# A kernel of attention and three MLP stages: X is turned for the token stage by VectorE and small transfers in place of TensorE

## The chip, the cores and the metric

The kernel runs on one core of a Trainium2 chip. The metric is the device time of one execution in microseconds (us). Engines are TensorE (PE), VectorE (DVE), ScalarE (ACT), GpSimd (POOL) and SyncE (SP), which here only issues transfers (DMA). SBUF is the on-chip memory of 128 partitions, PSUM the accumulators that PE writes; PE can't write SBUF.

## The reference, cut to what matters

There are 4 batches of S = 576 tokens with 512 features. Three stages follow one another:

```
x = attention(q, k, v)                       # 8 heads of 64, windowed and dilated masks
xk, xr = mu * x + (1 - mu) * x_prev          # feed-forward with token shift
x = sigmoid(xr @ w_r) * (relu(xk @ w_k)**2 @ w_v)
xt = x.transpose(0, 2, 1)                    # token mixer
u  = x + (relu(xt @ w_tok1) @ w_tok2).transpose(0, 2, 1)      # w_tok1 576x256
out = u + relu(u @ w_ch1) @ w_ch2            # channel mixer, w_ch1 512x1536
```

All matrices are float32. A product is made of three PE passes on two parts of each operand: hi (the value rounded to fp32r, by ACT) and lo (value minus hi, by DVE or POOL): hi*hi, lo*hi and hi*lo (lines 761 to 763).

## The kernel before, in words

Everything is kept with features on the partitions: `X` holds for each batch 4 blocks of 128 features, each 577 columns (tokens) wide, and is computed in phase 1 (attention and feed-forward, interleaved by tables of units: `ff[t]` is the list of steps of unit t, 20 units for each half batch, counted from the end with negative numbers). Phase 2 does the token mixer and the channel mixer, batch after batch.

The token mixer's first product, `token_up` (L1104), contracts over tokens, so it needs x with tokens on the partitions: `xT`, 5 tiles of 512 features, four of 128 tokens and a tail of 64 tokens, the tail written twice, to both halves of the partitions. `x_transpose` (L1061) makes it: for a tile, PE does 4 transposes by a product with `ident` (L1082) into a PSUM bank, ACT rounds the bank to `xT_hi` (L1093, L1094) and DVE subtracts to `xT_lo` (L1100, L1101). For batch 0 these steps stand in the last two half batches of the feed-forward, two units apart. For batches 1 to 3 they stand near the end of the channel mixer of the batch before, behind its last `channel_up` (`if i == len(seq)` in `phase2_body`), because `xT` shares its memory with `u`, the operand of `channel_up`. They read `xcur`, a copy of the batch's X that POOL requests (`load_x`, L1030).

In the channel mixer 24 steps (2 halves of 288 tokens, 12 blocks of 128 of the 1536) each do `channel_up` (12 matmuls into one of four `work` banks), ACT's `h_hi` and DVE's `h_lo`, and, two steps later, `channel_down` (12 matmuls into four accumulators). `ORDER` and `READ` say which of the four work banks a product gets and whose reading it must wait for. Output: `finish` adds, `out_blocks` (DVE, STREAM_TRANSPOSE, which turns each 32x32 block in place) and `store` (SP, 16 transfers of 32 partitions for each half batch, in runs of 32 floats).

Each engine executes its own list in order, and all waits are on semaphores. SP's list is: loads of q, k, v and weights; `load_token_weights`; `load_channel_weights`; then the stores of each batch.

## Time and profile before

| | before |
|---|---|
| median of 3 runs | 729.09 us (728.98 to 730.18) |
| the profiled execution's own time | 729.79 us |
| its span, first to last instruction | 728.0 us |
| PE, DVE, ACT, POOL busy | 715.6, 372.6, 255.9, 224.8 us |

PE is the engine with almost no idle time in any part. In a row of the timeline the first number is the start in us, the second the duration in us, then engine, line, operation, output<-input, shapes and how many instructions were merged; in square brackets stands the idle time before it and what ended that. Matmuls overlap in PE's pipeline, so the distance of their starts tells their price, not the duration.

### The profile page before, as it was taken

What the parts mean: (1) busy time and instruction counts of PE and PEld (TensorE: products, weight loads), DVE (VectorE), ACT (ScalarE), POOL (GpSimd) and SP (SyncE); (2) the same over time, 40 slices, a digit from 0 to 9 for tenths busy, and PEclk for the clock granted to TensorE, in tenths of its full rate; (3) what the DMA queues carried; (4) which work ended last, traced back from release to release, by engine and by line L of the source; (5) the groups of instructions that cost most, each with busy time, mean ns of one, the idle gap of its engine ahead of it and who ended that gap; (6) DMA issues with size and microseconds to landing.
All of it is one profiled execution on the core that took longest, in us unless ns stands there. A gap on an engine that the chain in (4) does not pass through costs nothing.

```text
span 728.0 us, 15646 instructions
## 1 busy us (share of the span) xinstructions
PE 715.6 (98%) x6463; PEld 691.6 (95%) x6463; DVE 372.6 (51%) x629; ACT 255.9 (35%) x628; POOL 224.8 (31%) x237
## 2 busy tenths in 40 slices
PE   8999999999999999999999999999999999999997
PEld 7778899999999999999999998999999999999997
DVE  6588877687777768576741224412244122451222
ACT  3585463635454453645431112311123111231111
POOL 5497664756464655734054000000000000000000
PEclk9999999999999999999999999999999999999999
DMA  9921333222322320201902011200103002010021
GB/s 210 295 60 31 53 72 69 48 56 50 73 39 50 66 41 20 70 1 36 375 2 66 6 29 19 80 1 1 33 14 85 1 1 33 9 25 1 1 34 33
DMA packets 127190, 39.89 MB, mean 55 GB/s; under 512 B 116168, under 2 KB 120720, under 8 KB 127120
## 3 DMA queue, kind: packets, MB, share of 16 engines
q1 hardware_dynamic: 122864, 33.39, 20.5%
q0 software_dynamic: 1088, 4.72, 1.9%
q10 hardware_dynamic: 3168, 0.79, 0.6%
q8 instruction: 51, 0.84, 0.5%
q14 instruction: 19, 0.16, 0.1%
HBM read 29.43 MB, written 4.72 MB: 47 GB/s over the span
## 4 chain that ended last, share of the span: by engine, by line
PE 90%; DVE 3%; POOL 2%; issue 1%; DMA 1%; ACT 1%; DVEq 0%; POOLq 0%; ACTq 0%
PE bank L761 12%; PE bank L763 11%; PE bank L762 11%; PE tq L761 8%; PE tq L762 8%; PE tq L763 8%; PE bank L1245 4%; PE bank L1244 4%; PE s L1245 4%; PE bank L1243 4%; PE s L1243 3%; PE s L1244 3%; PE bank L683 3%; PE s L549 2%; PE bank L647 1%
## 5 line engine op out<-in xcount | busy, mean ns | idle before, releaser
L1220 DVE SCALAR_TENSOR_TENSOR h_lo<-tq,h_hi 128x288 fp32r<-128x288 f32 x48 | 22.0, 457 | 114.1 <-ACT h_hi L1216 114.1
L1220 DVE SCALAR_TENSOR_TENSOR h_lo<-bank,h_hi 128x288 fp32r<-128x288 f32 x48 | 22.0, 458 | 113.4 <-ACT h_hi L1216 113.4
L881 DVE RECIPROCAL rg<-rg 128x288 f32<-128x288 f32 x32 | 61.2, 1919 | 3.0 <-ACT rg L870 3.0
L1216 ACT ACTIVATE h_hi<-tq 128x288 fp32r<-128x288 f32 x48 | 19.7, 411 | 122.3 <-PE tq L763 122.3
L1216 ACT ACTIVATE h_hi<-bank 128x288 fp32r<-128x288 f32 x48 | 19.7, 411 | 121.7 <-PE bank L763 121.7
L848 POOL TENSOR_TENSOR k_lo<-kr,k_hi 128x288 fp32r<-128x288 f32 x64 | 54.5, 857 | 24.8 <-ACT k_hi L844 23.9
L1035 POOL DMA_DIRECT2D xcur<-X x4 | 3.2, 798 | 180.4 <-DVE U L1162 163.8
L1245 PE MATMUL bank<-h_lo,C_hi 128*128 128x288 f32 x192 | 56.9, 296 | 0.0
L1244 PE MATMUL bank<-h_hi,C_lo 128*128 128x288 f32 x192 | 56.9, 296 | 0.0
L1243 PE MATMUL s<-h_hi,C_hi 128*128 128x288 f32 x192 | 56.9, 296 | 0.0
L1245 PE MATMUL s<-h_lo,C_hi 128*128 128x288 f32 x192 | 56.8, 296 | 0.0
L1243 PE MATMUL bank<-h_hi,C_hi 128*128 128x288 f32 x192 | 56.8, 296 | 0.0
L1244 PE MATMUL s<-h_hi,C_lo 128*128 128x288 f32 x192 | 56.7, 295 | 0.0
L761 PE MATMUL bank<-u_hi,C_hi 128*128 128x288 f32 x192 | 56.7, 295 | 0.0
L761 PE MATMUL tq<-u_hi,C_hi 128*128 128x288 f32 x192 | 56.6, 295 | 0.0
L762 PE MATMUL tq<-u_hi,C_lo 128*128 128x288 f32 x192 | 56.6, 295 | 0.0
L762 PE MATMUL bank<-u_hi,C_lo 128*128 128x288 f32 x192 | 56.6, 295 | 0.0
L763 PE MATMUL tq<-u_lo,C_hi 128*128 128x288 f32 x192 | 56.6, 295 | 0.0
L763 PE MATMUL bank<-u_lo,C_hi 128*128 128x288 f32 x192 | 56.6, 295 | 0.0
L761 PE MATMUL bank<-k_hi,WV_hi 128*128 128x288 f32 x184 | 55.8, 304 | 0.0
L762 PE MATMUL bank<-k_hi,WV_lo 128*128 128x288 f32 x184 | 54.3, 295 | 0.0
L763 PE MATMUL bank<-k_lo,WV_hi 128*128 128x288 f32 x184 | 54.1, 294 | 0.0
(215 smaller groups left out, 2241.1 us busy)
## 6 DMA issues: line engine op xcount, KB each, us to landing
C_raw<-in_moe_w_ch SPq DMA_DIRECT2D x6, 1024.0 KB, 11.6
xcur<-X POOLq DMA_DIRECT2D x4, 1152.0 KB, 5.8
out_x<-blocks SPq DMA_DIRECT2D x112, 36.0 KB, 1.7
vt<-in_v SPq DMA_DIRECT2D x40, 80.0 KB, 2.5
qraw<-in_q SPq DMA_DIRECT2D x128, 24.0 KB, 1.9
kraw<-in_k SPq DMA_DIRECT2D x128, 24.0 KB, 1.9
vt<-in_v SPq DMA_DIRECT2D x7, 320.0 KB, 3.4
WK_raw<-in_moe_w_k SPq DMA_DIRECT2D x4, 512.0 KB, 7.3
```

The costliest lines, as they stand in the source:

```text
L549: last = e.matmul(s2[64 * a:64 * a + 64, c0:c0 + KB], qT[rows, q0:q0 + 64], keys(rows, s, c), start=True, stop=True)
L683: last = e.matmul(o_[64 * h:64 * h + 64, SU * s + QB * c:SU * s + QB * (c + 1)], raw_v(n, slice(0, KB), 2 * s + h)[:, D * c:D * (c + 1)], ...
L761: e.matmul(out_ap, wh, xh, start=start and i == 0, stop=False)
L762: e.matmul(out_ap, wl, xh, start=False, stop=False)
L763: last = e.matmul(out_ap, wh, xl, start=False, stop=stop and i == len(kts) - 1)
L848: e.tensor_tensor(lo, t, hi.bitcast(F32), ALU.subtract).then_inc(Z.lo_done, 1)
L881: e.reciprocal(t, t).then_inc(Z.r_done, 1)
L1216: e.activation(hi, ps, ACT.Relu).then_inc(Z.h2h_done, 1)
L1220: e.scalar_tensor_tensor(lo, ps, 0.0, hi.bitcast(F32), ALU.max, ALU.subtract).then_inc(Z.h2l_done, 1)
L1243: e.matmul(o_, wh, xh, start=f == 0, stop=False)
L1244: e.matmul(o_, wl, xh, start=False, stop=False)
L1245: return e.matmul(o_, wh, xl, start=False, stop=f == FT2 - 1)
```

## The change

`x_transpose` is gone. In its place:

- `x_blocks(b, d)`: DVE turns the 32x32 blocks of feature block d of batch b in `X` into a buffer `xblocks` (one instruction for the four full token tiles, one for the tail). For b > 0 it waits for the stores of batch b - 2 and the copy of batch b - 1, since `xblocks` lies on memory that they read.
- `x_rows(b)`: SP issues 32 transfers from SBUF to SBUF that carry the blocks to their rows: 16 for the tail (32 partitions, 4 runs of 32 floats each; both halves of the partitions) and 16 for the main part (32 partitions, 16 runs of 32 floats). The result is `xraw`, x with tokens on the partitions, in float32. For b > 0 it waits for `xcur` of that batch.
- `x_parts(b, i)`: ACT and DVE split `xraw` from SBUF into `xT_hi` and `xT_lo`, tail first, one instruction each (`token_up` waits for the tail, and then tile by tile).
- `out_blocks` of half 0 waits until the transfers of the next batch have landed.
- The transposes leave `ORDER`, so the products get other banks (the order of products is the same).

In phase 1 the block transposes stand at units -30 to -27, the transfers at -26, the splits of the token weights at -25, -23 and -21 (before -26, -24, -22) and the splits of x at -16 to -8 (before -20 to -12). In phase 2 the block transposes of the next batch stand in steps 3 to 6, the transfers in step 6, the splits where the transposes stood.

```diff
--- before.py
+++ after.py
@@ -149,6 +149,10 @@
         T2, o = weights("T2", [P, 2 * S], o)
         xT, _ = split("xT", [P, NTT * DM], o)
         u, _ = split("u", [P, DT * S], o)
+        xraw0 = at("xraw0", [P, NTT * DM], F32, o + 4 * NTT * DM)
+        xblocks = [at("xblocks0", [P, DT * S], F32, o), at("xblocks1", [P, DT * S], F32, 0)]
+        xraw = at("xraw", [P, (NTT - 1) * DM], F32, 4 * DT * S)
+        xtail = xraw0[:, (NTT - 1) * DM:NTT * DM]
         o += 8 * NTT * DM
         assert base + o <= nc.sbuf_usable_end, (base + o, nc.sbuf_usable_end)
 
...
@@ -1039,9 +1043,9 @@
 
 
         ORDER = [("t2", i) for i in range(8)] + [("c1", i) for i in range(2 * FT2)] + \
-                [("x", i) for i in range(NTT)] + [("t1", i) for i in range(2)]
+                [("t1", i) for i in range(2)]
         TB = len(ORDER)
-        READ = {"x": (Z.xtl_done, NTT, 1), "t1": (Z.h1l_done, 3, 1), "t2": (Z.u_done, 8, 0), "c1": (Z.h2l_done, 2 * FT2, 0)}
+        READ = {"t1": (Z.h1l_done, 3, 1), "t2": (Z.u_done, 8, 0), "c1": (Z.h2l_done, 2 * FT2, 0)}
 
         def work_bank(b, kind, i):
             return work[(TB * b + ORDER.index((kind, i))) % 4]
@@ -1056,50 +1060,71 @@
             n = 2 * n if k == "t1" else n
             wait(e, s, per * (b + ahead) + n + 1)
 
-        XSEQ = [0, NTT - 1] + list(range(1, NTT - 1))
-
-        def x_transpose(b, i, first=False):
+        XS = DM // P * 4
+
+        def x_blocks(b, d):
+
+            dst = xblocks[b > 0]
+            main_, tail = dst[:, 0:XS * P], dst[:, XS * P:DT * S]
+
+            def vector(e):
+                if b == 0:
+                    e.wait_ge(Z.o_done, ND)
+                    e.wait_ge(Z.x2_done, 2 * DT)
+                else:
+                    e.wait_ge(Z.x2_done, DT * NU)
+                    e.wait_ge(Z.xc_in, 16 * b)
+                    for done in out_done:
+                        wait(e, done, OUT * (b - 1))
+                e.transpose(main_.rearrange("p (t d n) -> p d t n", d=DT, n=P)[:, d],
+                            xcols(b, d, 0, 4 * P).rearrange("p (t n) -> p t n", n=P)).then_inc(Z.xb_done, 1)
+                e.transpose(tail[:, 64 * d:64 * (d + 1)], xcols(b, d, 4 * P, 64)).then_inc(Z.xb_done, 1)
+            return dict(vector=vector)
+
+        XT_IN = 16 * 32
+
+        def x_rows(b):
+
+            src = xblocks[b > 0]
+            main_, tail = src[:, 0:XS * P], src[:, XS * P:DT * S]
+            raw = xraw if b else xraw0[:, 0:XS * P]
+
+            def sync(e):
+                e.wait_ge(Z.xb_done, 2 * DT * (b + 1))
+                if b:
+                    e.wait_ge(Z.xc_in, 16 * (b + 1))
+                for g in range(4):
+                    rows = slice(32 * g, 32 * (g + 1))
+                    for c in range(2):
+                        for r in (0, 64):
+                            e.dma_start(tiles(xtail[r + 32 * c:r + 32 * (c + 1), :], DT)[:, :, rows],
+                                        tiles(tail[rows, :], DT)[:, :, 32 * c:32 * (c + 1)]).then_inc(Z.xt_in, 16)
+                for g in range(4):
+                    rows = slice(32 * g, 32 * (g + 1))
+                    for c in range(4):
+                        e.dma_start(tiles(raw[32 * c:32 * (c + 1), :], XS)[:, :, rows],
+                                    tiles(main_[rows, :], XS)[:, :, 32 * c:32 * (c + 1)]).then_inc(Z.xt_in, 16)
+            return dict(sync=sync)
+
+        XSEQ = [NTT - 1] + list(range(NTT - 1))
+
+        def x_parts(b, i):
 
             n = NTT * b + i
             tt = XSEQ[i]
-            tail = tt == NTT - 1
-            nt = S - TT * tt if tail else P
-            ps = acc[i % 2] if first else work_bank(b - 1, "x", i)
-
...
+            c = slice(DM * tt, DM * (tt + 1))
+            raw = xtail if tt == NTT - 1 else (xraw if b else xraw0)[:, c]
+
+            def scalar(e):
+                e.wait_ge(Z.xt_in, XT_IN * (b + 1))
                 if i == 0:
                     wait(e, Z.c1p_done, 2 * FT2 * b)
-                if tail:
-                    e.activation(part(xT[0], nt), ps[0:nt, :], ACT.Copy)
-                e.activation(part(xT[0], 0), ps[0:nt, :], ACT.Copy).then_inc(Z.xth_done, 1)
+                e.activation(xT[0][:, c], raw, ACT.Copy).then_inc(Z.xth_done, 1)
 
             def vector(e):
                 e.wait_ge(Z.xth_done, n + 1)
...
+                e.tensor_tensor(xT[1][:, c], raw, xT[0][:, c].bitcast(F32), ALU.subtract).then_inc(Z.xtl_done, 1)
+            return dict(scalar=scalar, vector=vector)
 
         def token_up(b, m, first=False):
 
@@ -1120,7 +1145,7 @@
                     else:
                         e.wait_ge(Z.ptb_done, ND)
                         e.wait_ge(Z.x2_done, DT * NU - 1)
-                    e.wait_ge(Z.xtl_done, NTT * (b + 1))
+                    e.wait_ge(Z.xtl_done, NTT * b + 1)
                     e.wait_ge(Z.w_lo2, N_T)
                     t0 = DM * (NTT - 1)
                     for i, (w, x) in enumerate(((0, 0), (1, 0), (0, 1))):
@@ -1128,8 +1153,8 @@
                             r = slice(64 * m_, 64 * m_ + 64)
                             c0 = TOK * (NTT - 1) + P * m_
                             e.matmul(bank(m_)[:, :], T1[w][r, c0:c0 + P], xT[x][r, t0:t0 + DM], start=i == 0, stop=False)
-                product(e, bank(m)[:, :], T1, cols(TOK, P * m, P), xT, cols(DM, 0, DM), range(NTT - 1), start=False)\
-                    .then_inc(Z.t1p_done, 1)
+                product(e, bank(m)[:, :], T1, cols(TOK, P * m, P), xT, cols(DM, 0, DM), range(NTT - 1), start=False,
+                        before=None if m else lambda kt: e.wait_ge(Z.xtl_done, NTT * b + kt + 2)).then_inc(Z.t1p_done, 1)
 
             def scalar(e):
                 e.wait_ge(Z.t1p_done, 2 * b + m + 1)
@@ -1262,6 +1287,8 @@
                 e.wait_ge(Z.fin_done, 8 * b + 4 * h + d + 1)
                 if d == 0:
                     wait(e, out_done[h], OUT * b)
+                    if h == 0 and b < B - 1:
+                        e.wait_ge(Z.xt_in, XT_IN * (b + 2))
                 e.transpose(blocks[h][:, HALF * d:HALF * (d + 1)], U[:, S * d + HALF * h:S * d + HALF * (h + 1)])\
                     .then_inc(Z.ob_done, 1)
             return dict(vector=vector)
@@ -1313,7 +1340,7 @@
             return dict(scalar=scalar, vector=vector, sync=sync)
 
         def token_start(b, first=False):
-            return [x_transpose(b, tt, first) for tt in range(NTT)], [token_up(b, m, first) for m in range(2)]
+            return [x_parts(b, i) for i in range(NTT)], [token_up(b, m, first) for m in range(2)]
 
         def phase2_body(b, last=False):
 
@@ -1330,6 +1357,10 @@
             for i in range(len(seq) + 2):
                 if i < len(seq):
                     steps.append(channel_up(b, *seq[i]))
+                if not last and 3 <= i < 3 + DT:
+                    steps.append(x_blocks(nxt, i - 3))
+                if not last and i == 2 + DT:
+                    steps.append(x_rows(nxt))
                 if i == len(seq):
                     steps += xs
                 if i >= 2:
@@ -1351,11 +1382,15 @@
 
             xs, ups = token_start(0, first=True)
             ff = feed_forward_all()
-            behind = [[split_weights2(i)] for i in range(N_T)] + [[x] for x in xs]
             ff[-8].append(load_channel_weights())
             ff[-3].append(split_weights2(N_T))
-            for i, x in enumerate(behind):
-                ff[14 + 2 * i - 2 * UNITS] += x
+            for d in range(DT):
+                ff[d - 30].append(x_blocks(0, d))
+            ff[-26].append(x_rows(0))
+            for i in range(N_T):
+                ff[2 * i - 25].append(split_weights2(i))
+            for i, x in enumerate(xs):
+                ff[2 * i - 16].append(x)
             return prologue() + [load_token_weights()] + flat(ff) + \
                 [load_x(0), split_weights2(N_T + 1), split_weights2(N_C1), ups[0], ups[1], first_token_down(0),
                  split_w_ch2(1), split_weights2(N_2), split_w_ch2(2)]
```

How the queues change is shown at three places. The first is PE at the end of batch 0's channel mixer (lines of the two kernels differ by 25 there; `s` and `bank` are the accumulators of `channel_down`). Before:

```order
L1244 MATMUL bank<-h_hi,C_lo 128x288
L1245 MATMUL bank<-h_lo,C_hi 128x288
L1082 MATMUL bank<-ident,xcur 128x128 x4
L1082 MATMUL bank<-ident,xcur 64x128 x4
L1082 MATMUL tq<-ident,xcur 128x128 x8
L1082 MATMUL bank<-ident,xcur 128x128 x4
L1243 MATMUL s<-h_hi,C_hi 128x288
L1244 MATMUL s<-h_hi,C_lo 128x288
```

The same place of PE's list in the changed kernel:

```order
L1269 MATMUL bank<-h_hi,C_lo 128x288
L1270 MATMUL bank<-h_lo,C_hi 128x288
L1268 MATMUL s<-h_hi,C_hi 128x288
L1269 MATMUL s<-h_hi,C_lo 128x288
L1270 MATMUL s<-h_lo,C_hi 128x288
```

The 20 transposes are gone, and the product behind them follows at once.

The second is DVE near the end of the feed-forward (half batch 6: `rg` is the gate, `mixed` the mix of x for the next half, `T_lo` the token weights' lo). Before:

```order
L881 RECIPROCAL rg<-rg 128x288 x2
L907 TENSOR_TENSOR X<-tq,rg 128x288
L881 RECIPROCAL rg<-rg 128x288
L732 SCALAR_TENSOR_TENSOR mixed<-dif,mus,X 128x288
L307 TENSOR_TENSOR T_lo<-T_raw,T_hi 128x1024
L907 TENSOR_TENSOR X<-bank,rg 128x288
L732 SCALAR_TENSOR_TENSOR mixed<-dif,mus,X 128x288
L881 RECIPROCAL rg<-rg 128x288
```

In the changed kernel:

```order
L885 RECIPROCAL rg<-rg 128x288
L1079 STREAM_TRANSPOSE xblocks_121<-X 128x4x128
L1081 STREAM_TRANSPOSE xblocks_121<-X 128x64
L1079 STREAM_TRANSPOSE xblocks_121<-X 128x4x128
L1081 STREAM_TRANSPOSE xblocks_121<-X 128x64
L885 RECIPROCAL rg<-rg 128x288
L1079 STREAM_TRANSPOSE xblocks_121<-X 128x4x128
L1081 STREAM_TRANSPOSE xblocks_121<-X 128x64
L911 TENSOR_TENSOR X<-tq,rg 128x288
L1079 STREAM_TRANSPOSE xblocks_121<-X 128x4x128
L1081 STREAM_TRANSPOSE xblocks_121<-X 128x64
L885 RECIPROCAL rg<-rg 128x288
```

Two pairs of block transposes stand ahead of the second reciprocal and two behind it, and the token weights' lo goes behind the second mix.

The third is SP from the token weights to the first stores of the changed kernel (`C_raw` are the channel weights, `xblocks_121` and `xblocks_122` the two block buffers):

```order
L284 DMA T_raw<-in_moe_w_tok 128x2x576
L1100 DMA xraw_120<-xblocks_121 32x4x32 x16
L1105 DMA xraw_120<-xblocks_121 32x16x32 x16
L293 DMA C_raw<-in_moe_w_ch 128x4x512
L295 DMA C_raw<-in_moe_w_ch 128x4x512
L293 DMA C_raw<-in_moe_w_ch 128x4x512 x2
L295 DMA C_raw<-in_moe_w_ch 128x4x512 x2
L1100 DMA xraw_120<-xblocks_122 32x4x32 x16
L1105 DMA xraw<-xblocks_122 32x16x32 x16
L1303 DMA out_x<-blocks_104 32x9x32 x16
```

Before, the channel weights stand right behind the token weights, and the stores right behind the channel weights; now 32 transfers stand in front of each.

## Rows read from the trace of the kernel before

**Rows 1.** Page: busy time, granted clock in 40 slices, chain by engine

```profile
PE 715.6 (98%) x6463; PEld 691.6 (95%) x6463; DVE 372.6 (51%) x629; ACT 255.9 (35%) x628; POOL 224.8 (31%) x237
...
PEclk9999999999999999999999999999999999999999
...
PE 90%; DVE 3%; POOL 2%; issue 1%; DMA 1%; ACT 1%; DVEq 0%; POOLq 0%; ACTq 0%
```

**Rows 2.** Line 1082, on batch 0: count, ns min/median/max, first and last start

```profile
L1082 PE MATMUL s<-ident,X x20: 270/272/277, 322.4 to 337.3; 128*128 128x128 f32 x16, 128*64 128x128 f32 x4
```

**Rows 3.** Timeline of PE, feed-forward (start us, duration us, instruction)

```profile
322.39 0.60 PE L1082 MATMUL s<-ident,X 128*128 128x128 f32 x4
322.75 0.38 PE L761 MATMUL bank<-xk_hi,WK_hi 128*128 128x288 f32 x1
322.96 0.29 PE L762 MATMUL bank<-xk_hi,WK_lo 128*128 128x288 f32 x1
```

**Rows 4.** Timeline of PE, end of batch 0's channel stage

```profile
440.60 0.30 PE L1243 MATMUL s<-h_hi,C_hi 128*128 128x288 f32 x1
...
442.18 1.04 PE L1082 MATMUL bank<-ident,xcur 128*128 128x128 f32 x8
...
444.61 0.38 PE L1243 MATMUL s<-h_hi,C_hi 128*128 128x288 f32 x1
444.83 0.30 PE L1244 MATMUL s<-h_hi,C_lo 128*128 128x288 f32 x1
...
447.74 0.29 PE L1245 MATMUL bank<-h_lo,C_hi 128*128 128x288 f32 x1
448.10 0.46 PE L1130 MATMUL bank<-xT_hi,T_hi 64*128 64x512 f32 x1
```

**Rows 5.** Timeline of ACT, the same place

```profile
440.80 0.41 ACT L1216 ACTIVATE h_hi<-tq 128x288 fp32r<-128x288 f32 x1 [2.79 <-PE tq L763]
...
444.54 1.06 ACT L1094 ACTIVATE xT_hi<-tq 128x512 fp32r<-128x512 f32 x2
```

**Rows 6.** Timeline of DVE, the same place

```profile
441.24 0.46 DVE L1220 SCALAR_TENSOR_TENSOR h_lo<-tq,h_hi 128x288 fp32r<-128x288 f32 x1 [2.74 <-ACT h_hi L1216]
...
447.17 0.67 DVE L1101 TENSOR_TENSOR xT_lo<-bank,xT_hi 128x512 fp32r<-128x512 f32 x1
...
449.22 1.53 DVE L1265 STREAM_TRANSPOSE blocks<-U 128x288 f32<-128x288 f32 x4
```

**Rows 7.** Output stores: timeline of SP; line 1276 (ns), to landing (us)

```profile
449.71 9.24 SPq L1276 DMA_DIRECT2D out_x<-blocks  x16
...
L1276 SPq DMA_DIRECT2D out_x<-blocks x112: 315/455/1907, 416.7 to 704.6; - x112
...
DMA to landing us min/median/max: 1.5/1.7/3.2
```

**Rows 8.** One microsecond of the stores: PE, PEld, DVE, ACT, POOL, PEclk, DMA share, GB/s

```profile
451.00:452.00 1.00, 1.00 (x6) 0.84 (x5) 0.00 (x0) 0.00 (x0) 0.00 (x0) 1.00 0.45 74
```

**Rows 9.** The copy to xcur: timeline of POOL; its landing

```profile
389.64 0.77 POOL L1035 DMA_DIRECT2D xcur<-X  x1
...
DMA to landing us min/median/max: 5.6/5.8/9.0
```

**Rows 10.** Timeline of DVE, first output transpose of batch 0

```profile
416.17 0.47 DVE L1265 STREAM_TRANSPOSE blocks<-U 128x288 f32<-128x288 f32 x1
```

**Rows 11.** Timeline of DVE, feed-forward of half batch 6

```profile
304.42 3.77 DVE L881 RECIPROCAL rg<-rg 128x288 f32<-128x288 f32 x2 [2.97 <-ACT rg L870]
311.40 0.46 DVE L907 TENSOR_TENSOR X<-tq,rg 128x288 f32<-128x288 f32 x1 [3.21 <-PE tq L763]
...
319.00 1.06 DVE L732 SCALAR_TENSOR_TENSOR mixed<-dif,mus,X 128x288 f32<-128x288 f32 x1
```

**Rows 12.** Timeline of ACT, feed-forward of half batch 7

```profile
332.18 0.40 ACT L829 ACTIVATE kr<-tq 128x288 f32<-128x288 f32 x1
```

**Rows 13.** DVE subtraction with both operands in SBUF (count | busy us, mean ns)

```profile
L250 DVE TENSOR_TENSOR WV_lo<-WV_raw,WV_hi 128x512 fp32r<-128x512 f32 x4 | 5.3, 1337 | 3.7 <-ACT WV_hi L242 3.7
```

More of the change, by code:

```diff
@@ L171, in build @@
             wt_in c1_in0 c1_in1 c1_in2 c2_in0 c2_in1 c2_in2 w_hi2 w_lo2
-            xc_in xp_done t1p_done t2p_done c1p_done c1w_done c2w_done xth_done xtl_done h1h_done h1l_done u_done uh_done ul_done
+            xc_in xb_done xt_in t1p_done t2p_done c1p_done c1w_done c2w_done xth_done xtl_done h1h_done h1l_done u_done uh_done ul_done
             h2h_done h2l_done c2_done fin_done ob_done lt_done ra_done rv_done out_done0 out_done1""".split()
@@ L1063, in x_transpose @@
+        XSEQ = [NTT - 1] + list(range(NTT - 1))
+        def x_parts(b, i):
             n = NTT * b + i
             tt = XSEQ[i]
-            tail = tt == NTT - 1
-            nt = S - TT * tt if tail else P
-            ps = acc[i % 2] if first else work_bank(b - 1, "x", i)
-            def tensor(e):
-                if first:
-                    if i == 0:
-                        e.wait_ge(Z.masked, ND)
-                        e.wait_ge(Z.x2_done, DT * 2)
-                    elif i >= 2:
-                        e.wait_ge(Z.xtl_done, i - 1)
-                else:
-                    work_free(e, b - 1, "x", i)
-                    if i == 0:
-                        e.wait_ge(Z.xc_in, 16 * b + 16)
-                for d in range(DT):
-                    c0 = (XC * d if first else S * d) + TT * tt
-                    last = e.transpose(ps[0:nt, P * d:P * (d + 1)], (X if first else xcur)[:, c0:c0 + nt], ident[:, :])
-                last.then_inc(Z.xp_done, 1)
@@ L1085, in part @@
-            def part(t, r0):
-                return t[r0:r0 + nt, DM * tt:DM * (tt + 1)]
+            c = slice(DM * tt, DM * (tt + 1))
+            raw = xtail if tt == NTT - 1 else (xraw if b else xraw0)[:, c]
             def scalar(e):
-                e.wait_ge(Z.xp_done, n + 1)
+                e.wait_ge(Z.xt_in, XT_IN * (b + 1))
                 if i == 0:
                     wait(e, Z.c1p_done, 2 * FT2 * b)
-                if tail:
-                    e.activation(part(xT[0], nt), ps[0:nt, :], ACT.Copy)
-                e.activation(part(xT[0], 0), ps[0:nt, :], ACT.Copy).then_inc(Z.xth_done, 1)
+                e.activation(xT[0][:, c], raw, ACT.Copy).then_inc(Z.xth_done, 1)
@@ L1096, in vector @@
             def vector(e):
                 e.wait_ge(Z.xth_done, n + 1)
-                hi = part(xT[0], 0).bitcast(F32)
-                if tail:
-                    e.tensor_tensor(part(xT[1], nt), ps[0:nt, :], hi, ALU.subtract)
-                e.tensor_tensor(part(xT[1], 0), ps[0:nt, :], hi, ALU.subtract).then_inc(Z.xtl_done, 1)
-            return dict(tensor=tensor, scalar=scalar, vector=vector)
+                e.tensor_tensor(xT[1][:, c], raw, xT[0][:, c].bitcast(F32), ALU.subtract).then_inc(Z.xtl_done, 1)
```

## The prediction

> **What bounds the kernel now.** I read the summary of the page first: PE is busy for 715.6 of 728.0 us, and the chain that ended last lies for 90% on PE; the granted clock is at its upper level (2.4 GHz) in all 40 slices [rows 1]. So whatever leaves PE's queue shortens the run by its pitch there, as long as nothing that PE waits for comes later, and no other engine's load matters by its sum. Then the line of the transposes: 80 of them, 4 for each of 5 token tiles of 4 batches; 20 (batch 0) read `X` inside the feed-forward [rows 2], the other 60 read `xcur`, in blocks of 20 at the end of a channel stage. Their listed 272 ns is a latency in a pipelined engine, so I take starts from the timeline instead, and then ask, stretch by stretch, what follows them on ACT and DVE and who would be late.
>
> **What goes from PE.** Twelve matmuls of a channel product take 440.60 to 442.18, a pitch of 0.132 us [rows 4].
> - Feed-forward, batch 0: the four transposes start at 322.39, and the second matmul behind them at 322.96 [rows 3]. Without them that distance is one pitch: 0.57 - 0.13 = 0.44 us, five times: 2.2 us.
> - Batches 1 to 3: from 442.18 to 444.83, the second matmul behind the block of 20 [rows 4]: 2.65 - 0.13 = 2.52 us, three times: 7.6 us.
> - `token_up` starts 0.36 us behind the last channel matmul (447.74 to 448.10, rows 4), 0.23 over the pitch. DVE's last `xT_lo` ended at 447.17 + 0.67 = 447.84 [rows 6], so part of it is a wait for the splits; I take 0.1 of it as won, three times 0.3 us (bounds 0 and 0.7).
> Gross: 2.2 + 7.6 + 0.3 = 10.1 us.
>
> **What takes their place at the end of a channel stage.** The ups end at 440.60, and three downs of 12 matmuls follow (3 x 1.58). Without transposes `token_up` would start at 440.60 + 4.74 = 445.3 instead of 448.1. The splits still can't start before the last up, because `xT` lies on `u`. ACT's last `h_hi` starts at 440.80, and its `xT_hi` pieces of 512 columns run at 0.53 us each in a burst [rows 5]: the first ends at 441.8, the fifth at 444.0. DVE follows at 0.67 us a piece [rows 6]: the tail, which is now the first, is ready at 442.5 and the fifth at about 445.2. So even the last piece is there when PE comes, and the new waits tile by tile ask for it only 3 us later. Cover: PE work of three downs; lost cover costs 0.67 us per piece that DVE is late. Behind them DVE has four `finish` and four output transposes (1.53 us for four, rows 6), which had nearly 2 us of idle time behind them. Cost 0.
> The four STREAM_TRANSPOSEs of 512 columns and four of 64 per batch: four of 288 take 1.53 us, 0.38 each [rows 6], so about 0.62 + 0.15 us a pair, 3.1 us a batch. In batches 1 to 3 each pair stands behind one `h_lo`, and DVE idles 2.7 us before each of these [rows 6]. Cost 0.
>
> **The transfers.** Per batch SP issues 32 of them: 16 of the tail (16 KB, 128 runs of 128 B) and 16 of the main part (64 KB, 512 runs). The trace has no SBUF-to-SBUF transfer of such runs. Nearest row: the output stores, 36 KB in 288 runs of 128 B. An issue takes 0.455 us in the median and up to 1.9, sixteen take 9.24 us with their waits for DVE (0.58 each), and a transfer lands 1.7 us after its issue [rows 7]. I take 0.54: 32 x 0.54 + 1.7 = 19.0 us from first issue to last landing. Lower end 32 x 0.455 + 1.7 = 16.3. During the stores the 16 engines are busy for 0.45 and move 74 GB/s [rows 8], that is 12.5 ns a run; 512 runs over 16 engines would be 0.40 us, under the issue. Upper end: 36 KB per 0.455 us is 79 GB/s out of 32 partitions, and if that were a limit of such a quarter, 64 KB would take 0.83 us: 16 x 0.83 + 16 x 0.54 + 1.7 = 23.6 us. I take 19, since the engines' 0.45 says that the issue sets the pace there.
> The Trainium skill (SBUF — State Buffer, Door 1: The DMA port swizzle) says that partitions 0 to 31 reach 8 of the 16 DMA ports; by its 436 GB/s for all ports 64 KB would take about 0.3 us (an estimate from that page), and the issue would set the pace, as in my value. The rows don't contradict it, but show only 79 GB/s.
>
> **Where their end is waited for.** There are two kinds of place.
> (a) Batch 0, in the feed-forward. The fourth pair of block transposes stands behind DVE's product with `rg` at 311.40 [rows 11], so SP starts at about 312.6 and the last transfer lands at 331.6. ACT asks for it at its first `xT_hi`, just ahead of the `kr` piece that it now evicts at 332.18 [rows 12]. Three of the five groups of transposes (1.3 us) lie before this place, so ACT gets there at about 330.5 and waits about 1 us. PE fills that bank again two products (3.2 us) after the product's end, at about 333.8; ACT's `xT_hi` and `kr` and DVE's `xT_lo` and square need about 1.9 us after the landing. PE so loses landing + 1.9 - 333.8, nothing at 19.0 us, and whatever a landing is above 19.3 us: 4.3 us at the upper end.
> (b) The store's block transpose of batch b on DVE now waits for the transfers of batch b + 1. For batch 1 these start only once POOL's `xcur` copy, issued at 389.64, has landed 5.8 us later [rows 9], here 393.3 (2.1 us are gained before it); with 19.0 us that is 412.3, and DVE asks at 416.17 [rows 10], here 414.1. Behind the waiting transpose DVE's next `h_lo` is queued, which PE needs two steps later; PE loses only above about 27.5 us. For batches 2 and 3 the copy is early, and the margin is about 10 us larger.
>
> **DVE ahead of batch 0's transfers.** The reciprocals from 304.42 on leave DVE idle for 3.21 us before 311.40 [rows 11], just the length of the four pairs, but they are spread in front of and behind the second reciprocal, and the token weights' splits move one unit later, between mixes. Playing the new order through with the old durations, the `mixed` piece of 319.00 [rows 11] comes 1 to 1.5 us later, and from it ACT's and POOL's parts, which PE needs within 3 us. Bounds 0 and 1.5 us; I take 0.5, since most of the shift is inside the slack.
> One row speaks against the change here: DVE's subtraction of 128 x 512 takes 0.67 us with a PSUM operand and POOL idle [rows 6], and 1.337 us where both operands are in SBUF and POOL works [rows 13]; the five `xT_lo` of batch 0 change from the one to the other. That is up to 3.3 us more on DVE, spread over nine units with 2 to 3 us of idle; it costs PE nothing unless the landing is late too, and is a part of the 4.3 us. The Trainium skill (SBUF — State Buffer, SBUF: two separate sides) has this as a rule: a VectorE operation with two SBUF inputs and a GpSimd operation lock each other out for whole instructions. By it the five would each wait out a POOL instruction; without it the term is 0. In batches 1 to 3 POOL is idle, so both give 0.
>
> **Sum.** 10.1 - 0.5 = 9.6 us. The profiled execution took 729.79 us, 1.79 over its span; it would take 720.2 (span 718.4). The median of the runs before is 729.09, 0.7 lower, so I forecast 719.5 us.
>
> **Rivals.**
> 1. *Transfers late in the feed-forward.* They take 21 to 24 us, ACT stalls with `kr` behind it, and PE loses 2 to 4.5 us once. For it: PE's margin is 0.3 us at my value, a single issue can take 1.9 us. Against: the median issue is 0.455. Time 721.5 to 724.
> 2. *DVE or the splits bound.* The pieces of `xT` come later than PE in batches 1 to 3, or DVE's work before the feed-forward's last half costs its full 1.5 us. For: one piece late at each end is 0.67, three times 2; with the 1.5, 3.5 less 0.5: about 722.5. Against: 445.2 against 445.3 and waits tile by tile.
> 3. *Slower than before: the transfers set the pace of the stages.* If a main transfer runs on few engines, or a run costs far over 12.5 ns, (a) and (b) both stall: PE loses (T - 19.3) + (T - 27.5), with T the time of 32. It decides from T = 28.5 us, 0.84 us per transfer on average, where the first alone is 9.6. At T = 32: 12.7 + 4.5 = 17.2 us, 729.09 - 9.6 + 17.2 = 736.7 us. Against: the stores' engines are at 0.45.
> 4. *The change does not shorten PE.* The new waits could hold PE where the transposes stood; it would need 2.5 us at each end, more than the 445.2 can explain: 728 to 730.
>
> **How the numbers follow.** Forecast 0.66 (718.7 to 721), rivals 1 and 2 together 0.25, rival 3 0.06, rival 4 0.03. The range reaches from all bounds of the small terms in favour (0.4 more from the waits, 0.5 of DVE kept: 718.6) to rival 1's end, 724. Below 0.2% (1.5 us) this kernel's runs tell no difference; of the cases, 0.91 lie faster by more, 0.03 within, 0.06 slower.
>
> **What would show it.** Right: no PE rows on `ident` with `xcur` or `X`; the second matmul behind each such place one pitch on; `token_up` in batches 1 to 3 within 0.3 us of the last down; SP's 32 issues in 15 to 19 us; ACT's first `xT_hi` of batch 0 waiting about 1 us for a DMA with PE unbroken; the store's block transpose without a wait for a DMA. Wrong: PE idle after about 332 us released by `kr`; a DMA wait on DVE at its first output transposes; transfers over 0.8 us apart; PE waiting for `xT_lo` at 445.

## The result and the profile after

The changed kernel takes 727.15 us (median of 9 runs, 726.54 to 728.28) against 729.39 of the kernel before beside it (728.66 to 730.18): ratio 0.9971, 95% interval [0.9961, 0.9981]. It is 2.2 us faster, where 9.6 were forecast. The profiled execution took 727.52 us, span 725.7.

Line numbers move: the block transposes are L1079 and L1081, the transfers L1100 (tail) and L1105 (main), ACT's `xT_hi` L1122, DVE's `xT_lo` L1126; L761 to L763 are now L765 to L767, L1243 to L1245 now L1268 to L1270. The page first, as in [rows 1]:

```profile
PE 709.1 (98%) x6383; PEld 685.2 (94%) x6383; DVE 382.0 (53%) x657; ACT 253.3 (35%) x624; POOL 225.2 (31%) x237
...
PE   8989999999999999997999999999999999999997
...
PEclk9999999999999999998999999999999999999999
...
PE 85%; SPq 6%; DVE 2%; POOL 2%; issue 2%; DMA 1%; ACT 1%; DVEq 0%; ACTq 0%
```

The 80 transposes are gone from PE. In one slice (number 19, 327 to 345 us) the granted clock fell, and 6% of the chain that ended last now lies on SP's queue: about half of that is the loads of the first 26 us, the rest the new transfers from 313.47 on. The waits of PE name the place:

```profile
PE tq L765 <- DVE kr L837: 3.8, 1, 3.8
```

(total us, times, longest). Follow it backwards from the timelines. First SP's issues of batch 0, and in a fence of their own the two lines of transfers with the stores beside them (issue in ns, min/median/max), which answer to [rows 7]:

```profile
313.47 10.76 SPq L1100 DMA_DIRECT2D xraw<-xblocks  x16
324.27 11.58 SPq L1105 DMA_DIRECT2D xraw<-xblocks  x16
```

```profile
L1100 SPq DMA_DIRECT2D xraw<-xblocks x64: 585/601/1610, 313.5 to 583.0; - x64
...
L1105 SPq DMA_DIRECT2D xraw<-xblocks x64: 601/629/1518, 324.3 to 594.3; - x64
...
L1303 SPq DMA_DIRECT2D out_x<-blocks x112: 315/455/2027, 424.9 to 702.3; - x112
```

An issue of such a transfer takes 0.60 or 0.63 us in the median, not 0.455, the next one starts 0.04 us behind its end, and with a few long ones (the longest of batch 0 takes 1.5 us) the 32 need 22.4 us. ACT asks for them at 331.65 and waits 5.66 us, with `kr` behind it (first fence, ACT); DVE waits for ACT (second):

```profile
337.31 0.63 ACT L1122 ACTIVATE xT_hi<-xraw 128x512 fp32r<-128x512 f32 x1 [5.66 <-DMA xraw<-xblocks]
337.85 0.39 ACT L833 ACTIVATE kr<-tq 128x288 f32<-128x288 f32 x1
```

```profile
337.98 0.69 DVE L1126 TENSOR_TENSOR xT_lo<-xraw,xT_hi 128x512 fp32r<-128x512 f32 x1 [6.43 <-ACT xT_hi L1122]
338.58 0.45 DVE L837 SCALAR_TENSOR_TENSOR kr<-tq,kr 128x288 f32<-128x288 f32 x1
```

And PE, whose bank that `kr` holds, stops between two matmuls:

```profile
335.00 0.29 PE L767 MATMUL bank<-xk_lo,WK_hi 128*128 128x288 f32 x1
339.09 0.61 PE L765 MATMUL tq<-xr_hi,WR_hi 128*128 128x288 f32 x1 [3.80 <-DVE kr L837]
339.50 0.44 PE L766 MATMUL tq<-xr_hi,WR_lo 128*128 128x288 f32 x1
339.74 0.44 PE L767 MATMUL tq<-xr_lo,WR_hi 128*128 128x288 f32 x1
...
344.54 0.44 PE L766 MATMUL bank<-xr_hi,WR_lo 128*128 128x288 f32 x1
344.78 0.36 PE L767 MATMUL bank<-xr_lo,WR_hi 128*128 128x288 f32 x1
344.98 0.29 PE L765 MATMUL bank<-xr_hi,WR_hi 128*128 128x288 f32 x1
345.11 0.29 PE L766 MATMUL bank<-xr_hi,WR_lo 128*128 128x288 f32 x1
```

The stop is 4.09 us where a pitch is 0.13: 3.96 lost. Then look at the starts, not at the waits: from 339.50 on they are 0.24 us apart, from 344.98 on 0.13 again. No wait is written at any of these rows. The windows say why (PE, PEld, DVE, ACT, POOL, granted clock, DMA share, GB/s):

```profile
333.00:334.00 1.00, 1.00 (x10) 1.00 (x9) 0.00 (x0) 0.00 (x0) 0.38 (x1) 1.00 0.39 60
...
338.00:339.00 1.00, 0.00 (x0) 0.00 (x0) 1.00 (x3) 0.87 (x3) 0.35 (x1) 0.54 0.00 0
341.00:342.00 1.00, 1.00 (x6) 1.00 (x6) 0.30 (x1) 0.00 (x0) 0.60 (x1) 0.50 0.00 0
344.00:345.00 1.00, 1.00 (x7) 1.00 (x6) 0.76 (x1) 0.21 (x1) 0.56 (x1) 0.54 0.00 0
345.00:346.00 1.00, 1.00 (x9) 1.00 (x9) 1.00 (x2) 0.79 (x2) 0.00 (x0) 1.00 0.00 0
```

During the stop the granted clock fell to its lower level (1.2 GHz), and the 24 matmuls behind the stop ran at half speed: from 339.09 to the first product with `WV` (348.17) it is 9.08 us, where the kernel before needs 6.38 (6.82 less its 0.44 of transposes). The stop brought 2.70 us more with it. The Trainium skill (TensorE: Matmul & The Clock Gate, Part 1: The HAM clock gate) has both halves of this: the gate knows two levels only, and an idle TensorE comes back at the lower one. The trace agrees: 0.50 and 1.00, with 0.54 only in the microseconds in which it changes. The stops of 1.0 to 1.7 us in e2 and e10 below left it at 1.00.

The 2.70 us belong to this execution. Its fall lasted 6.8 us (five microseconds at 0.50 and two at 0.54), and its mean granted clock is 0.994. Four of the nine runs have a mean of 0.997, which leaves room for about 4.4 us at the lower level in all (an estimate: 0.003 of 725 us, at half speed). They took 726.64 to 727.15 us, the other five 726.54 to 728.28 with a median of 727.89. So the fall must have been shorter in these four, and what it costs is no constant.

Two other places. In the feed-forward the mixes came late, and PE waited for POOL's part of one. The same product before took 1.59 us and ended where [rows 3] begins; here it takes 2.31:

```profile
322.73 0.30 PE L766 MATMUL bank<-xk_hi,WK_lo 128*128 128x288 f32 x1
322.87 0.29 PE L767 MATMUL bank<-xk_lo,WK_hi 128*128 128x288 f32 x1
323.44 0.40 PE L765 MATMUL bank<-xk_hi,WK_hi 128*128 128x288 f32 x1 [0.28 <-POOL xk_lo L755]
```

With some shorter irregular pitches that is 0.72 us more. On DVE's side the mix was late for two reasons: the block transposes had pushed the reciprocals back, and DVE took a 1.7 us split of the token weights (317.07) ahead of its reciprocal (318.70) and the mix (320.56). And in batch 1 DVE waits for the transfers at the first output transpose, with PE unbroken, while at the end of that channel stage DVE's five splits and PE's step from the last down to `token_up` are as forecast [rows 4, 6] (DVE, then PE):

```profile
424.36 0.48 DVE L1292 STREAM_TRANSPOSE blocks<-U 128x288 f32<-128x288 f32 x1 [2.58 <-DMA xraw<-xblocks]
...
447.29 3.10 DVE L1126 TENSOR_TENSOR xT_lo<-xraw,xT_hi 128x512 fp32r<-128x512 f32 x5
```

```profile
450.77 0.29 PE L1270 MATMUL bank<-h_lo,C_hi 128*128 128x288 f32 x1
451.00 0.51 PE L1155 MATMUL bank<-xT_hi,T_hi 64*128 64x512 f32 x2
```

Setting the same instructions of both traces side by side gives the balance of the spans (after less before, us):

| place | us |
|---|---|
| attention and first half batches, up to 284.7 us (the same code; this part differs by up to 2.1 us between the profiles) | +0.83 |
| late mixes | +0.72 |
| transposes gone from the feed-forward, 5 x 0.44 | -2.2 |
| PE stopped by `kr` | +3.96 |
| matmuls at the lower clock | +2.70 |
| a wait for `xcur` grew shorter (this stretch varies by 0.9 us between profiles) | -0.53 |
| batches 1 to 3: 2.59, 2.63, 2.60 | -7.8 |
| sum (spans: 725.7 - 728.0) | -2.3 |

### The profile page after: what moved, and what is told of

Read it like the earlier page. It is cut to its first block, busy times and chain, and to the rows that moved or that the text cites. A ratio compares the mean times of both kernels' runs of the same rounds, so it can differ in the third digit from the quotient of the medians.

```text
span 725.7 us, 15662 instructions
## 1 busy us (share of the span) xinstructions
PE 709.1 (98%) x6383; PEld 685.2 (94%) x6383; DVE 382.0 (53%) x657; ACT 253.3 (35%) x624; POOL 225.2 (31%) x237
## 4 chain that ended last, share of the span: by engine, by line
PE 85%; SPq 6%; DVE 2%; POOL 2%; issue 2%; DMA 1%; ACT 1%; DVEq 0%; ACTq 0%
PE bank L765 11%; PE bank L766 11%; PE bank L767 11%; PE tq L765 8%; PE tq L767 8%; PE tq L766 8%; PE bank L1270 4%; PE bank L1269 4%; PE s L1270 4%; PE bank L1268 4%; PE s L1268 4%; PE s L1269 4%; PE bank L687 3%; SPq L372 2%; PE s L553 2%
## 5 line engine op out<-in xcount | busy, mean ns | idle before, releaser
L1245 DVE SCALAR_TENSOR_TENSOR h_lo<-tq,h_hi 128x288 fp32r<-128x288 f32 x48 | 22.0, 458 | 109.6 <-ACT h_hi L1241 109.6
L1245 DVE SCALAR_TENSOR_TENSOR h_lo<-bank,h_hi 128x288 fp32r<-128x288 f32 x48 | 21.9, 457 | 106.4 <-ACT h_hi L1241 106.4
L852 POOL TENSOR_TENSOR k_lo<-kr,k_hi 128x288 fp32r<-128x288 f32 x64 | 54.4, 854 | 29.5 <-ACT k_hi L848 28.5
L1270 PE MATMUL bank<-h_lo,C_hi 128*128 128x288 f32 x192 | 57.0, 297 | 0.0
L1270 PE MATMUL s<-h_lo,C_hi 128*128 128x288 f32 x192 | 56.8, 296 | 0.0
L1268 PE MATMUL bank<-h_hi,C_hi 128*128 128x288 f32 x192 | 56.8, 296 | 0.0
L765 PE MATMUL bank<-u_hi,C_hi 128*128 128x288 f32 x192 | 56.6, 295 | 0.0
L765 PE MATMUL tq<-u_hi,C_hi 128*128 128x288 f32 x192 | 56.6, 295 | 0.0
L1268 PE MATMUL s<-h_hi,C_hi 128*128 128x288 f32 x192 | 56.6, 295 | 0.0
L767 PE MATMUL bank<-u_lo,C_hi 128*128 128x288 f32 x192 | 56.5, 294 | 0.0
L767 PE MATMUL tq<-u_lo,C_hi 128*128 128x288 f32 x192 | 56.5, 294 | 0.0
L765 PE MATMUL bank<-k_hi,WV_hi 128*128 128x288 f32 x184 | 55.8, 303 | 0.0
L767 PE MATMUL bank<-k_lo,WV_hi 128*128 128x288 f32 x184 | 54.1, 294 | 0.0
```

Of the source, the lines that this page charges most:

```text
L765: e.matmul(out_ap, wh, xh, start=start and i == 0, stop=False)
L767: last = e.matmul(out_ap, wh, xl, start=False, stop=stop and i == len(kts) - 1)
L852: e.tensor_tensor(lo, t, hi.bitcast(F32), ALU.subtract).then_inc(Z.lo_done, 1)
L1245: e.scalar_tensor_tensor(lo, ps, 0.0, hi.bitcast(F32), ALU.max, ALU.subtract).then_inc(Z.h2l_done, 1)
L1268: e.matmul(o_, wh, xh, start=f == 0, stop=False)
L1270: return e.matmul(o_, wh, xl, start=False, stop=f == FT2 - 1)
```

## The experiments

The theory: only the transfers of batch 0 are late; the stop and the clock behind it cost 6.7 us, the late mixes 0.7, and all other terms stand. In `phase1` the number in `ff[...]` is the half batch's step at which a piece of work is put. Each edit is against the changed kernel.

| kernel | us, median (range) | ratio to before, 95% interval |
|---|---|---|
| e1 splits of `xT` at -10 | 720.44 (720.18 to 721.56) | 0.9883 [0.9868, 0.9898] |
| e2 the same at -14 | 721.63 (721.23 to 722.71) | 0.9901 [0.9885, 0.9918] |
| e3 30 filler matmuls | 726.28 (725.95 to 726.68) | 0.9960 [0.9945, 0.9975] |
| e4 batch 0 on PE as before | 721.80 (721.16 to 722.02) | 0.9897 [0.9882, 0.9912] |
| e5 15 filler matmuls | 724.91 (724.19 to 725.68) | 0.9939 [0.9922, 0.9955] |
| e6 e1, token splits later | 719.79 (719.14 to 720.14) | 0.9866 [0.9851, 0.9881] |
| e7 transfers earlier | 719.77 (718.88 to 720.62) | 0.9866 [0.9852, 0.9881] |
| e8 e1, rows' step later | 719.34 (719.23 to 720.07) | 0.9863 [0.9848, 0.9878] |
| e9 e6 and e7 together | 719.70 (718.99 to 720.67) | 0.9865 [0.9840, 0.9889] |
| e10 e1, blocks 4 steps later | 723.65 (722.61 to 724.22) | 0.9918 [0.9890, 0.9945] |
| e11 e1, blocks 3 steps later | 719.75 (719.54 to 719.98) | 0.9866 [0.9839, 0.9893] |

**e1: ask for the transfers later.**

```
-                ff[2 * i - 16].append(x)
+                ff[2 * i - 10].append(x)
```

> Batch 0's five splits of x move six units later in the feed-forward (units -10 to -2 in place of -16 to -8); nothing else changes. Theory A (the loss is ACT's wait of 5.7 us for the transfers at the first split, which stops PE for 3.97 us and drops its granted clock to the lower level for 24 matmuls, 2.7 us more): both vanish, 727.15 - 6.7 = 720.4 us, with no PE idle released by kr and the clock at its upper level through 300 to 350. Theory B (the loss is DVE's or SP's work as such and only moves): PE is stopped elsewhere near the end of the feed-forward, 723 to 727 us.

720.44 us. SP's issues are the same, but no instruction of ACT waits for them, PE isn't stopped by `kr`, and over 50 us (300 to 350) the clock is 1.00 and PE busy for 49.7:

```profile
300.00:350.00 50.00, 49.71 (x395) 49.12 (x394) 35.38 (x46) 25.34 (x54) 19.66 (x24) 1.00 0.41 112
```

The changed kernel has 45.92 and 0.93 there. So the loss of 6.7 us (6.4 by the ratios) hangs on where ACT stands in its list when the transfers land.

**e2: ask a little later.** The same line with -14.

> The five splits of batch 0 move only two units later (-14 to -6). Theory A: PE comes 3.2 us later to the bank that it waits for, so it is stopped for about 0.8 us in place of 3.97. If the clock drop belongs to long stops, it is gone: 720.4 + 0.8 = 721.2 us; if any stop brings it, 723.9 us. Theory B: no change from 727.15 beyond 1 us.

721.63 us, and the short stop is seen: 0.91 us over the pitch, without a fall of the clock.

```profile
338.27 0.40 PE L765 MATMUL bank<-xr_hi,WR_hi 128*128 128x288 f32 x1 [0.74 <-DVE kr L837]
```

e1 and e2 together with the changed kernel say that a stop of 0.9 us costs about itself (1.2 us in the medians) and one of 4 us costs 1.7 times itself.

**e3 and e5: keep PE at work during the stop.** Products of the identity into an unused part of a bank, ahead of the stopped product; the transfers stay late.

```
+        def stall_cover(n):
+            def tensor(e):
+                e.wait_ge(Z.x_done, ND)
+                for _ in range(n):
+                    e.matmul(o_ps[:, 384:384 + P], ident[:, :], ident[:, :], start=True, stop=True)
+            return dict(tensor=tensor)
...
+            ff[-13].append(stall_cover(30))      # e5: 15
```

> Splits stay at -16; 30 matmuls of 128x128 on the constant identity (about 3.3 us of PE, result unused) are put on PE right in front of the product that is stopped. Theory A: they fit into the stop of 3.97 us, the stop stays, the clock stays at its upper level behind it: 727.15 - 2.7 = 724.5 us. If the lower clock costs nothing by itself, or is not a consequence of the stop, the time stays at 727.2; if the stop is not there in the timed runs, it rises by up to 3.3.

726.28 us. Each such matmul of full fp32 appears as two records, so the filler is 6.86 us long, not 3.3, and eats what it gives:

```profile
334.10 6.86 PE L934 MATMUL bank<-ident 128*128 128x128 f32 x60
```

The clock stays at 1.00 and the products behind it take 6.46 us instead of 9.08, but as a time this run tells nothing. So half of it:

> As e3_warm with 15 matmuls in place of 30, since each came as two passes of 0.11 us there and the 30 took 6.6 us: now 3.3 us, inside the stop of 3.97 us. Theory A (the lower clock follows from PE's stop and costs 2.7 us): clock at the upper level behind it, the four gate products in 6.4 in place of 9.1 us, 727.15 - 2.7 = 724.5 us. If the clock drop is no cost of its own: 727.2.

724.91 us, 2.2 less than the changed kernel, with the same late transfers (ACT waits 6.5 us) and PE still waiting for the rest:

```profile
333.84 3.51 PE L934 MATMUL bank<-ident 128*128 128x128 f32 x30
338.64 0.40 PE L765 MATMUL tq<-xr_hi,WR_hi 128*128 128x288 f32 x1 [1.29 <-DVE kr L837]
```

From here the products take 6.50 us. The stopped product starts 4.93 us behind the last one ahead of the filler, no less than the 4.09 of the changed kernel, and still the time went down by 2.2 of the table's 2.7: the clock's fall is a cost by itself, beside the stop.

**e4: batch 0 by PE, batches 1 to 3 by transfers.** `x_first(i)`, the old transposes with their splits, takes the place of `x_parts` in batch 0; its block transposes and transfers are left out, and the three waits that count them go down by one batch.

```
-            return [x_parts(b, i) for i in range(NTT)], [token_up(b, m, first) for m in range(2)]
+            return [x_first(i) if first else x_parts(b, i) for i in range(NTT)], [token_up(b, m, first) for m in range(2)]
```

> Only batch 0 goes back to transposes on PE (with the old places of its steps and of the token weights' splits); batches 1 to 3 keep block transposes and transfers. Theory A: the gain of batches 1 to 3 stands alone: 729.39 - 3 x 2.6 = 721.6 us (721.1 if the 0.5 us at the first channel product is part of it). Theory B (transfers in batches 1 to 3 cost something too): 723 or more. DVE should still wait about 2 to 3 us for the transfers at its first output transpose of batch 0, with PE unbroken.

721.80 us, 7.2 less than the 728.97 beside it, and by the spans of the profiles (719.9 and 728.0) 8.1 less; three batches of 2.6 are 7.8. The 1.4 and 2.1 us from here down to e1 and e9 are batch 0's share, against the 2.2 forecast (e1 still has the late mixes, for which 0.5 was taken); e8 below shows how little a difference of 1 us says. DVE's first output transpose waits 4.0 us for the transfers here, again with PE unbroken.

**e6: the late mixes.** e1, and

```
-                ff[2 * i - 25].append(split_weights2(i))
+                ff[2 * i - 19].append(split_weights2(i))
```

> e1_splits_late with the three splits of the token weights six units later too (-19, -17, -15 in place of -25, -23, -21), so that they no longer stand between DVE's mixes for the last half batch. Theory (the 0.7 us at the first product of the last half batch is the 1024-column split and its wait for ACT, ahead of a reciprocal): PE has no idle time released by xk_lo, 720.44 - 0.7 = 719.7 us. Rival (it is the block transposes' 0.8 us): 720.3.

719.79 us, and PE no longer waits for `xk_lo`. From the product with that wait to the first one with `WV` it takes 19.51 us where e1 takes 19.91, so the trace vouches for 0.4 us: 0.6 at the mixes, less 0.2 given back in the products behind. The intervals of e1 and e6 overlap.

**e7: start the transfers earlier.** All block transposes of batch 0 at -32, the transfers at -31, the splits where the change had put them.

```
-                ff[d - 30].append(x_blocks(0, d))
-            ff[-26].append(x_rows(0))
+                ff[-32].append(x_blocks(0, d))
+            ff[-31].append(x_rows(0))
```

> Splits at -16 as in the changed kernel, but batch 0's block transposes two units earlier (all at -32, in DVE's idle 3 us ahead of the first reciprocal) and the transfers at -31. Theory A (only the landing against ACT's demand counts): the first issue moves from 313.5 to about 305.3, the last landing from 337.3 to about 329.3, ahead of ACT's 331.7, so stop and clock drop vanish: 720.4 us, 719.7 if the mixes gain as well. Rival (the transfers take longer beside the token weights' loads, or the stop has another cause): 722 or more.

719.77 us. Here the 32 issues take 21.5 us, the last lands before ACT asks, and the stop is gone:

```profile
305.30 10.74 SPq L1100 DMA_DIRECT2D xraw<-xblocks  x16
316.08 10.70 SPq L1105 DMA_DIRECT2D xraw<-xblocks  x16
```

It is the same cause mended from the other side: the time of the 32 is nearly the same and their start 8.2 us earlier. The wait for `xk_lo` is gone here too (the stretch of e6 takes 19.32 us), though the token weights' split still stands ahead of the reciprocal: the block transposes, now early, were as much its cause as the split.

**e8: transfers of batches 1 to 3 later.** e1 with `x_rows` at step 10 instead of 6.

> e1_splits_late with the transfers of batches 1 to 3 at step 10 of the channel stage in place of step 6. The output's first block transpose on DVE (step 15) then waits about 24.1 - 5 x 3.2 = 8 us for them in each of three batches. My term (b) says that PE loses only what exceeds about 6.7 us: 1.4 us each, 4.2 in all, 724.6 us, with a drop of the clock perhaps on top (up to 2.7 each). Rival (a wait of DVE there reaches PE at once, as 2.6 us seemed not to): 8 us each, 744. Rival (more cover than I thought): 720.4.

719.34 us, and it missed its purpose: `x_rows` is work of SP alone, SP's list has nothing between these two places, so SP issued as soon as the blocks and `xcur` were there (392.59; in e1 393.65). It is a second look at e1, and tells that two kernels whose engines have the same work in the same order stand 1.1 us apart in their medians; in the profiles 1.2 us of difference are there before any of the changed code (SP's first load of token weights at 300.38 and 301.58). e6 and e7 were measured beside e8 and are no faster than it, so their 0.65 and 0.67 us over e1 are no gain that the times show.

**e11 and e10: move what SP waits for.** e1, with the block transposes and `x_rows` three and four channel steps later.

```
-                if not last and 3 <= i < 3 + DT:
-                    steps.append(x_blocks(nxt, i - 3))
-                if not last and i == 2 + DT:
+                if not last and 6 <= i < 6 + DT:      # e10: 7
+                    steps.append(x_blocks(nxt, i - 6))   # e10: 7
+                if not last and i == 5 + DT:           # e10: 6
```

> As the kernel with the late splits (720.4), with the block transposes of batches 1 to 3 and the transfers behind them three channel steps (9.6 us) later. The last block transpose ends at about 396.2 in batch 1, SP starts 0.6 later, the last landing is 24.4 us on, at 421.2, and DVE's first output transpose, which asks at 414.5, waits about 6.5 us in each of the three batches instead of 2.6, 0 and 0. By the prediction's term (PE loses nothing until the landing is 6.7 us behind the ask) that is hidden: 720.2 to 721.0. Rival (PE has no such margin, each microsecond on DVE beyond one step of 3.2 us is lost): 3 x 3.3 = 9.9 us more, 730.

719.75 us. DVE waits 6.64, 6.11 and 4.91 us at its first output transpose of batches 1 to 3, and PE runs through.

> The same with four channel steps (12.8 us) instead of three: landing at about 424.4, DVE waits about 9.7 us in each of three batches. By the prediction's term PE loses 9.7 - 6.7 = 3.0 us three times, 9 us: 729.5. If a stop of 3 us brings the granted clock down as the one of 3.97 us did, 2.7 us more each time: 737.5. Between the two if the clock falls for fewer than 24 matmuls. Rival (the margin is larger, since more than one bank stands between DVE and PE): 720.4, no stop of PE. The kernel with three steps and this one together place the point from which the transfers set the pace.

723.65 us. DVE waits 9.12, 8.44 and 8.73 us, and now PE stops, three times (DVE, then PE):

```profile
423.00 0.48 DVE L1292 STREAM_TRANSPOSE blocks<-U 128x288 f32<-128x288 f32 x1 [9.12 <-DMA xraw<-xblocks]
```

```profile
423.88 0.41 PE L1268 MATMUL s<-h_hi,C_hi 128*128 128x288 f32 x1 [1.40 <-DVE h_lo L1245]
...
514.63 0.41 PE L1268 MATMUL s<-h_hi,C_hi 128*128 128x288 f32 x1 [0.71 <-DVE h_lo L1245]
...
605.62 0.40 PE L1268 MATMUL s<-h_hi,C_hi 128*128 128x288 f32 x1 [1.01 <-DVE h_lo L1245]
```

Start to start these are 1.57, 0.88 and 1.16 us over a pitch, 3.6 together, and the medians differ by 3.9. Each DVE wait less its stop gives 7.55, 7.56 and 7.57 us: the margin is one number, below which a wait costs nothing and above which it costs itself. The expectation of 9 us was too high because it had the margin at 6.7 and the waits at 9.7; its rivals (no margin, a far larger one) fall. None of these stops brought the clock down.

**e9: both repairs of the feed-forward, together.** The edits of e6 and e7.

> Everything that paid alone, together: batch 0's block transposes and transfers at the half batches -32 and -31, the token weights' splits at -19, -17, -15, the pieces of xT from -10 on. Theory (the late landing with the clock behind it, and the late mixes, were the whole loss): nothing is left of either, so the time is at the level of the two best so far less a few tenths: 719.0 to 719.8, against 719.8 for each of the two alone. Rival (something else in the feed-forward is worth more than 0.5 us): below 718.8. Rival (the edits disturb one another, DVE's list filling up between the half batches -31 and -26): above 720.3.

719.70 us. There is no wait of ACT for the transfers and none of PE for the mixes, and the gains of e6 and e7 do not add: each had taken away the wait for the mixes by itself. e1, e6 to e9 and e11 all lie between 719.3 and 720.4, which is what is to be had from this change: 1.3% less than before.

## Why the prediction was wrong

The step that failed is the time of the transfers, "I take 0.54: 32 x 0.54 + 1.7 = 19.0 us". Measured: 22.4 us of issues and 2.1 from the last one to its landing less its own length, 23.8 us, 0.70 an issue. It is just beyond the 23.6 that was the upper bound (which should read 23.3: 0.455 us for 36 KB gives 0.81 us for 64 KB, not 0.83).

- *The row that it was read from.* The stores [rows 7] have the same bytes per run, but go to HBM; their issue takes 0.455 us in the median. Both forms of the new transfers take 0.60 to 0.63. That is not a matter of bytes or runs: 16 KB in 128 runs and 64 KB in 512 differ by 28 ns, and the upper bound, built on a limit by bytes (0.83 for the main part, 0.54 for the tail), came near the sum by chance. "The issue sets the pace" was right, and its size for this kind of transfer was in no row. What makes it longer was not tried.
- *Its consequence (a).* The start was forecast at 312.6 and was 313.47, the landing at 331.6 and was 337.3. ACT asked at 331.65, not at 330.5, and PE would have come to its bank at 335.1, not at 333.8, so the stop is 337.3 + 1.8 - 335.1 = 4.0 us; the rule "PE loses what landing is above 19.3 us" gives 4.5 us for 23.8. The mechanism, ACT's `xT_hi` with `kr` behind it, then DVE, then PE's bank, is that of rival 1, and e1, e2 and e7 show it from both ends.
- *The term that was missing.* Rival 1 was priced at 721.5 to 724 with PE losing the stop alone. The clock's fall behind it, 2.70 us in the profiled execution, stood in no term, and no reason was given for taking it as nothing; e5 shows it apart. With both, and 0.2 more for the mixes, the forecast would have been 719.5 + 3.96 + 2.70 + 0.2 = 726.4; the median is 0.8 above that, less than e1 and e8 stand apart.
- *Chances.* Rivals 1 and 2 had 0.25 together, for a value that stood on a guess between two ends. The margin of 0.3 us between T = 19.0 and the point where PE begins to lose was written down, and should have turned the case: with ends at 16.3 and 23.6, more than half of that span lay beyond it.

What held:

- *Gross gain.* 0.44 us five times; 2.59, 2.63 and 2.60 us per batch against 2.62 (2.52 and 0.1 of the waits). `token_up` starts 0.23 us behind the last down, 0.1 over the pitch; DVE's five splits there take 3.10 us, 0.62 each, and rival 2's first half and rival 4 fall.
- *DVE ahead of batch 0's transfers.* 0.5 taken, 0.72 measured, by the wait of PE for `xk_lo`. Both causes that the prediction names were at work: moving the token weights' split ends the wait (e6), and so does moving the block transposes (e7).
- *The block transposes.* 0.62 and 0.15 us taken; 0.70 and 0.20 in the median, 0.57 to 0.63 and 0.12 to 0.13 from start to start, at no cost in the batches.
- *xT_lo of batch 0 with both operands in SBUF.* 0.69, 0.87, 0.87, 0.69 and 0.63 us instead of 0.67, where up to 1.337 [rows 13] was feared: 0.4 us in all. The Trainium skill (SBUF — State Buffer, SBUF: two separate sides) has the later of two such instructions on VectorE and GpSimd wait until the other one is over. The two of 0.87 started while a subtraction of POOL had about 0.3 us left (340.07 against 340.39, 344.24 against 344.57) and took 0.2 us longer, the other three met practically none: that goes the same way, but is no test of the rule.
- *(b) and rival 3.* A wait of DVE at its first output transpose was called a sign against the forecast; it came (2.58 us), and was harmless as the working said. The margin behind the ask was put at 6.7 us and is 7.56, so in batch 1 the transfers would set the pace from T of about 28.4 us (20.9 us from SP's start at 393.65 to DVE's ask at 414.5 in e1, and 7.56), not 27.5. At 23.8 us rival 3 was far off, and e10 shows that it exists. (By its own terms rival 3 reaches the gain of 9.6 at T = 28.2, and its first term alone at 28.9; the 28.5 of the prediction is neither.)

With the cause gone the forecast stands: 719.3 to 720.4 against 719.5, with a span of 718.5 in e1 against 718.4. That it is met to a few tenths is luck, since the same work twice gave 1.1 us of difference (e1, e8).

## What to carry to other kernels

A bound on a transfer should come from a row with the same kind of source and destination; where there is none, ask first how late it may land, and if that point lies inside the bounds, move the work that asks, or the start, before arguing over the size: here one number in a list of steps was worth 6.7 us. A wait that stands in an in-order list costs whatever is queued behind it, but only beyond the margin of the buffers (0 for 6.6 us, 1.57 for 9.12), so measure that margin. When PE stops for microseconds, look at the granted clock behind the stop and count the half-speed matmuls as part of its price.

## What the runs showed of the hardware

- SP's issue of an SBUF-to-SBUF transfer: 0.60 us (128 runs of 128 B) and 0.63 us (512 runs), landing 1.8 and 2.1 us; of an SBUF-to-HBM store of 288 such runs 0.455 and 1.7. During the 16 transfers of 512 runs each (325 to 337 us) the 16 engines were busy for 0.39 to 0.72 of a microsecond, and moved 60 to 121 GB/s.
- A stop of PE of 4.09 us was followed by 24 matmuls at 0.24 us in the profiled execution, and, by the estimate from the mean clock, by fewer in four of the nine runs; stops of up to 1.7 us (e2, e10) by none. Lengths between these were not tried.
- A matmul of the fp32 identity by itself, 128 x 128, is two records in the trace, 0.114 to 0.117 us each.
